# First token blocks' low parts moved to GpSimd and eight steps later, and three smaller moves around them

## The reference

```
# q, k, v: (4 batches, 8 heads, 576 rows, 64)
scores = q @ k.T / 8, masked where row//64 < column//64
x = softmax(scores) @ v                    # as 2304 tokens x 512
x = (sigmoid(x @ w_gate) * (x @ w_val)) @ w_out      # 512 -> 1536 -> 512
p = domain_probs / (domain_probs.sum(-1) + 1e-9)
out = sum over e of p[:, e] * (relu(x @ w1[e]) @ w2[e])   # 4 experts, 512 -> 1024 -> 512
```

## Time and profile before

| | |
|---|---|
| median of 3 runs | 1469.93 us (1467.77 to 1473.21) |
| the profiled execution | 1468.38 us |
| its span | 1466.6 us |
| busy: TensorE, VectorE, ScalarE, GpSimd | 1418.0, 905.8, 728.5, 424.0 us |
| scores of step 0 begin | 14.36 us |
| last steps' row maxima | up to 281 us |

### The profile page before, as it was taken

How to read it: one execution, slowest core, us unless ns; L and a number is a source line. 1 busy time by engine, 2 the same in 40 slices (tenths; PEclk the granted TensorE clock), 3 DMA queues, 4 the chain that set the end, 5 groups by cost and what they waited for, 6 DMA issues and landing times.

```text
span 1466.6 us, 22252 instructions
## 1 busy us (share of the span) xinstructions
PE 1418.0 (97%) x7816; PEld 1288.6 (88%) x7816; DVE 905.8 (62%) x1557; ACT 728.5 (50%) x1472; POOL 424.0 (29%) x665
## 2 busy tenths in 40 slices
PE   6999988899999999999999999999999999999999
PEld 4777776799998989898999989899899999899897
DVE  4888879777646446376774546364857746364453
ACT  4878777666434334254663534253546535253341
POOL 3656655544302122021441112021134312021200
PEclk9999999999999999999999999999999999999999
DMA  7787797223214121122223132131222322131302
GB/s 177 182 205 179 188 225 174 60 66 87 81 35 144 44 86 59 57 87 86 65 81 100 60 100 65 51 95 45 77 87 72 98 61 72 44 101 43 97 12 79
DMA packets 201150, 136.76 MB, mean 93 GB/s; under 512 B 66096, under 2 KB 170576, under 8 KB 201040
## 3 DMA queue, kind: packets, MB, share of 16 engines
q1 hardware_dynamic: 200976, 135.31, 33.2%
q0 software_dynamic: 64, 0.04, 0.1%
HBM read 97.55 MB, written 9.44 MB: 73 GB/s over the span
## 4 chain that ended last, share of the span: by engine, by line
PE 84%; DVE 8%; DMA 2%; issue 2%; ACT 1%; SPq 1%; POOL 1%; ACTq 0%; DVEq 0%; POOLq 0%
PE pb L903 26%; PE pb L905 25%; PE pb L904 25%; PE pt L395 3%; PE ov L420 2%; DVE ptl L330 2%; DVE nmax L308 1%; PE st L432 1%; PE st L383 1%; DMA craw<-in_moe_w_dram 1%; PE st L384 1%; DVE x1p L343 1%; DMA xb<-x1d 1%; DVE qtl L336 1%; DVE ktl L336 1%
## 5 line engine op out<-in xcount | busy, mean ns | idle before, releaser
L903 PE MATMUL pb<-xch,ul 128*128 128x384 f32 x1176 | 398.9, 339 | 5.7 <-DVE cb L837 4.2
L905 PE MATMUL pb<-xch,uh 128*128 128x384 f32 x1176 | 393.5, 335 | 0.0
L904 PE MATMUL pb<-xcl,uh 128*128 128x384 f32 x1176 | 393.3, 334 | 0.0
L697 POOL TENSOR_TENSOR us<-ura 128x256 f32<-128x256 f32 x84 | 62.3, 742 | 851.4 <-DVE ul L659 833.2
L903 PEld LDWEIGHTS pb<-xch,ul 128*128 128x128 f32 x1176 | 220.7, 188 | 23.8 <-issue 16.7
L905 PE MATMUL pb<-ch,rh 128*128 128x512 f32 x576 | 224.6, 390 | 0.0
L904 PE MATMUL pb<-cl,rh 128*128 128x512 f32 x576 | 224.5, 390 | 0.0
L903 PE MATMUL pb<-ch,rl 128*128 128x512 f32 x576 | 224.0, 389 | 0.0
L904 PEld LDWEIGHTS pb<-xcl,uh 128*128 128x128 f32 x1176 | 220.9, 188 | 0.4
L905 PEld LDWEIGHTS pb<-xch,uh 128*128 128x128 f32 x1176 | 220.7, 188 | 0.0
L806 DVE TENSOR_TENSOR cl<-craw,ch 128x512 fp32r<-128x512 f32 x132 | 92.0, 710 | 114.4 <-ACT ch L741 114.0
(11 more groups left out here) (99 smaller groups left out, 2558.2 us busy)
## 6 DMA issues: line engine op xcount, KB each, us to landing
ura<-in_moe_w_dram SPq DMA_DIRECT2D x96, 256.0 KB, 3.1
craw<-in_moe_w_dram SPq DMA_DIRECT2D x96, 256.0 KB, 2.8
ura<-in_moe_w_gate_dram SPq DMA_DIRECT2D x36, 256.0 KB, 3.2
ura<-in_moe_w_val_dram SPq DMA_DIRECT2D x36, 256.0 KB, 3.2
craw<-in_moe_w_out_dram SPq DMA_DIRECT2D x36, 256.0 KB, 3.1
qhl<-qth SPq DMA_DIRECT2D x32, 144.0 KB, 2.7
qhl<-qtl SPq DMA_DIRECT2D x32, 144.0 KB, 2.6
qlh<-qtl SPq DMA_DIRECT2D x32, 144.0 KB, 2.6
```

Of the source, the lines that this page charges most:

```text
L697: nc.gpsimd.tensor_tensor(us[:, 0, :], a21, a22, ALU.add).then_inc(us_ok, 1)
L903: nc.tensor.matmul(acc, lhs[1], rhs[0], start=start, stop=False, skip_group_check=True)
L904: nc.tensor.matmul(acc, lhs[0], rhs[1], start=False, stop=False, skip_group_check=True)
L905: return nc.tensor.matmul(acc, lhs[0], rhs[0], start=False, stop=stop, skip_group_check=True)
```

## The change

Four things change, all inside the attention's span.

1. At the start, ScalarE and no longer SyncE issues the loads of k's first pair and the four stacked copies of k for pair 0.
2. The four GpSimd sums of weight units 0 and 1 stand in four steps (58 to 61, 78 to 81) and no longer all in step 60 or 80; `lo_s` for these two units becomes two operations of 512 columns, in steps 69 and 70, 87 and 88.
3. The token blocks' sums and high parts of f = 0 begin eight steps later (wait for xb in step 122 and no longer 114).
4. The 14 low parts of f = 0 are made by GpSimd (steps 126 to 149) and no longer by VectorE. Two of VectorE's in-place sums in each column half now wait for x_lo, the count of low parts made, before they overwrite a block (`sum_t`, i = 0 and 2).

In the diff, functions that only get an `eng` argument are left out (`load`, `stack`, `stack_k`, `x_minus`, `lo_b11`, `lo_t1`, `lo_b22`, `lo_t`; `x_dve_b21` becomes `lo_b21`).

```diff
 @block.sync
-            load(0, q_v, qn, q_in)
-            load(0, k_v, kn, k_in)
-            load(0, v_v, vn, v_in)
+            load(sp, 0, q_v, qn, q_in)
+            load(sp, 0, v_v, vn, v_in)
             next_q(0)
+            sp.wait_ge(prep_lo, 1)
             for h in range(2):
-                sp.wait_ge(prep_lo, 1)
                 stack_q(0, h)
-                sp.wait_ge(prep_lo, 2)
-                stack_k(0, h)
             next_k(0)
 @block.scalar
+            load(act, 0, k_v, kn, k_in)
             for p in range(2):
                 prep(p)
+            act.wait_ge(prep_lo, 2)
+            for h in range(2):
+                stack_k(act, 0, h)
             for t in range(STEPS + TAIL):
...
         def sum_t(f, c, i):
             if i == 0:
+                if f == 0:
+                    dve.wait_ge(x_lo, 2 * c + 1)
                 nc.vector.tensor_tensor(block_of(c, 0, 0), block_of(c, 1, 1), xt[:, c, :], ALU.subtract)\
...
             if i == 2:
                 dve.wait_ge(x_sum, XSUMS * f + 2 + 3 * c + 1)
+                if f == 0:
+                    dve.wait_ge(x_lo, 4 + 5 * c + 1)
                 nc.vector.tensor_tensor(block_of(c, 1, 0), block_of(c, 1, 0), block_of(c, 0, 0), ALU.subtract)\
...
+        def lo_s_half(n, m):
+            r = n % 2
+            at = slice(3 + 2 * m, 5 + 2 * m)
+            dve.wait_ge(ws_hi, n + 1)
+            lo = nc.vector.tensor_tensor(ul[r][:, at, :, :]..., us[:, 2 * m:2 * m + 2, :]..., uh[r][:, at, :, :]..., ALU.subtract)
+            if m == 1:
+                lo.then_inc(ws_lo, 1)
...
         def with_pool(pool, t):
-            if t == 60:
-                sums_of_weights(pool, 0)
+            if t in (58, 59, 60, 61):
+                sum_of_weights(pool, 0, t - 58)
...
+            if t in (126, 130):
+                lo_b11(pool, 0, (t - 126) // 4)
+            if t in (128, 132):
+                lo_t1(pool, 0, (t - 128) // 4)
+            for c in range(2):
+                first = 133 + 9 * c
+                if t == first:
+                    lo_b21(pool, 0, c)
+                if t == first + 2:
+                    lo_t(pool, 0, c, 0)
+                if t == first + 3:
+                    lo_b22(pool, 0, c)
+                if t in (first + 5, first + 7):
+                    lo_t(pool, 0, c, (t - first - 3) // 2)
         def with_act(act, t, qk_ps):
-            if t in (116, 118):
-                hi_b11(0, (t - 116) // 2)
+            if t in (123, 125):
+                hi_b11(0, (t - 123) // 2)
...
         def with_dve(dve, t, qk_ps):
-            if t in (114, 115):
-                sum_t1(0, t - 114)
+            if t in (122, 123):
+                sum_t1(0, t - 122)
...
+                if t == 129 + 8 * c:
+                    sum_t(0, c, 0)
+                if t == 130 + 8 * c:
+                    sum_t(0, c, 1)
+                if t == 135 + 9 * c:
+                    sum_t(0, c, 2)
```

More of the change, by code:

```diff
@@ L134, in x1_head, with load, stack @@
             return x1p[64 * (g % 2):64 * (g % 2) + 64, g // 2 % X1_RING, :]
+        def load(eng, n, src, dst, got):
+            for h in range(2):
+                eng.dma_start(dst[:, 0:4, h, :], src[2 * n + h, 0:4 * P, :]
+                              .rearrange("(t p) d -> p t d", p=P)).then_inc(got, 16)
+            eng.dma_start(dst[0:S - 4 * P, 4, :, :],
+                          src[2 * n:2 * n + 2, 4 * P:S, :].rearrange("a p d -> p a d")).then_inc(got, 16)
+        def stack(eng, moves, h, got):
+            for dst, at, src in moves:
+                dst = dst[at:at + 64, h, FRAME - S:FRAME] if dst.shape[2] == FRAME else dst[at:at + 64, h, :]
+                eng.dma_start(dst.bitcast(F32), src[64 * h:64 * h + 64, :].bitcast(F32)).then_inc(got, 16)
@@ L136, in _, with stack_k @@
+        def stack_k(eng, u, h):
+            stack(eng, ((khl[u], 0, kth), (khl[u], 64, ktl)), h, k_stacked[u][h])
         @block.sync
         def _(sp):
[L138 to L148, removed]
             def stack_q(u, h):
-                stack(((qhl[u], 0, qth), (qhl[u], 64, qtl), (qlh[u], 0, qtl), (qlh[u], 64, qth)), h, q_stacked[u][h])
-            def stack_k(u, h):
-                stack(((khl[u], 0, kth), (khl[u], 64, ktl)), h, k_stacked[u][h])
+                stack(sp, ((qhl[u], 0, qth), (qhl[u], 64, qtl), (qlh[u], 0, qtl), (qlh[u], 64, qth)), h,
+                      q_stacked[u][h])
@@ L156, in next_q @@
             def next_q(n):
                 sp.wait_ge(prep_ps, 2 * n + 1)
-                load(n + 1, q_v, qn, q_in)
+                load(sp, n + 1, q_v, qn, q_in)
             def next_k(n):
                 sp.wait_ge(prep_ps, 2 * n + 2)
-                load(n + 1, k_v, kn, k_in)
+                load(sp, n + 1, k_v, kn, k_in)
             def pair_out(n):
@@ L179, in pair @@
                 for h in range(2):
-                    stack_k(n % 2, h)
+                    stack_k(sp, n % 2, h)
                 after(sp, v_lo, CHUNKS * n)
-                load(n, v_v, vn, v_in)
+                load(sp, n, v_v, vn, v_in)
                 if not last:
@@ L620, in x_dve_rest @@
                 sum_t(f, c, i)
[L621 to L624, removed]
+            lo_t(dve, f, c, 0)
+            lo_b22(dve, f, c)
+            lo_t(dve, f, c, 1)
+            lo_t(dve, f, c, 2)
         def hi_a(act, n):
@@ L688, in load_xb, with sum_of_weights @@
             sp.dma_start(xb[:, :, :], x1d[:, :, SUPER * s:SUPER * s + SUPER]).then_inc(xb_in, 16)
-        def sums_of_weights(pool, n):
+        def sum_of_weights(pool, n, i):
             r = n % 2
[L692 to L702, removed]
+            a11, a12, a21, a22 = (ura[r][:, m, :] for m in range(4))
+            if i == 0:
+                pool.wait_ge(u_in[r], 32 * (n // 2 + 1))
+                if n:
+                    pool.wait_ge(ws_lo, n)
+                pool.sem_inc(pool_on, 1)
+                nc.gpsimd.tensor_tensor(us[:, 0, :], a21, a22, ALU.add).then_inc(us_ok, 1)
+            if i == 1:
+                nc.gpsimd.tensor_tensor(us[:, 2, :], a11, a21, ALU.subtract).then_inc(us_ok, 1)
+            if i == 2:
+                pool.wait_ge(us_ok, 4 * n + 1)
+                nc.gpsimd.tensor_tensor(us[:, 1, :], us[:, 0, :], a11, ALU.subtract).then_inc(us_ok, 1)
+            if i == 3:
+                pool.wait_ge(us_ok, 4 * n + 3)
+                nc.gpsimd.tensor_tensor(us[:, 3, :], a12, us[:, 1, :], ALU.subtract).then_inc(us_ok, 1)
         later = ExitStack()
@@ L1058, in with_act @@
                     hi_b22(0, c)
-                if t in (first + 5, first + 6, first + 7):
-                    hi_t(0, c, t - first - 5)
+                if t == 131 + 10 * c:
+                    hi_t(0, c, 0)
+                if t == 132 + 10 * c:
+                    hi_t(0, c, 1)
+                if t == 138 + 8 * c:
+                    hi_t(0, c, 2)
             k = t - STEPS
@@ L1212, in _ @@
             for n in range(2, UNITS * SUPERS):
-                sums_of_weights(pool, n)
+                for i in range(4):
+                    sum_of_weights(pool, n, i)
         @block.scalar
```

83 lines of the change are left out of this document (36 added, 47 removed).

## The result

The changed kernel takes 1475.11 us in the median of 12 runs (1474.09 to 1479.3), the kernel before 1470.2 of 12. The ratio is 1.0036 (95% interval 1.0025 to 1.0047): 5.3 us slower, where 1465, with 1457 to 1471, had been forecast. The profiled execution took 1479.3 (span 1477.5), 4.2 above the median and the slowest of the twelve, so that its waits can be longer than those of a usual one. TensorE's first product of the next stage starts at 292.50 instead of 283.13; what comes after takes 1.5 us more, in code that is the same. That part takes 1181.6 to 1186.5 us in the profiles of all versions here, so 1.5 us of it say nothing.

What follows compares the result with a forecast made beforehand. TensorE and VectorE, handing each other work in a ring, were taken to bound the attention, TensorE alone what follows. Start 1.2, weight sums 1.5 and token blocks 1.1 took 3.8 us off 1468.4; forecast 1465, range 1457 to 1471.

Steps and rivals of the forecast that it cites:

- eight steps are 12.2 us, so this wait goes: Token blocks: starting eight steps later ends VectorE's 3.49 us wait for the xb load.
- terms 4 to 6: Token blocks: VectorE's remaining sums cost 1.3 and 0.9 us, ScalarE's roundings 0.6, GpSimd and VectorE holding each other up 0.8.
- The start: Before the first score: ScalarE issuing k's loads and copies wins 1.2 us, ends nothing and 2.1; SyncE's issues set the time.
- rival C: Start: k's loads delay q's first load and the DMA engines are the limit; 0 instead of 1.2, 1466 us; chance 0.12.
- The weight sums: Steps 65 to 94: spread sums and halved subtractions win 1.5 us (0.5 to 2.5); other three halves and splits put at 2.5.
- step 70's 0.65: Weight units: the half subtraction at step 70, at a group's start where VectorE has no gap, costs its 0.65 us.
- The two new waits: Token blocks, steps 135 and 144: VectorE waits 3.2 and 4.4 us for GpSimd's low parts, 0.94 already a gap; sum 6.7.
- GpSimd's price: Token blocks: one low part of 384 columns takes GpSimd about 0.95 us, ends 0.73 and 1.46.
- The clock: Token blocks: the granted clock falls after each of two new waits, 1.3 us each, 2.6 together.
- The signs: VectorE waiting some 3 us at steps 135 and 144, clock 0.5 after each, no xb wait, first score 13.2, low parts 0.95.
- Rival A: Token blocks: low parts at 0.73, two waits of 2.0 us, clock stays; 6.4 won there, 1459 us; chance 0.26.
- Rival B: Steps 130 to 149: GpSimd becomes the bound and normalisations come late; 10 us lost there, 1476 us; chance 0.08.

Runs made afterwards that it cites:

- a_late: Changed kernel with VectorE's third sums three steps later, other second-half sums and ScalarE's roundings shifted too, GpSimd's work unchanged: 1464.65 us, ratio 0.9967.
- a_lows_dve: Changed kernel with the 14 low parts moved back from GpSimd to VectorE at the same steps: 1470.63 us, ratio 1.0003.
- a_late_early: Changed kernel with VectorE's sums later and three quarters of the xb load issued in four earlier pieces: 1460.61 us, ratio 0.9941.
- b_start: Kernel before with the start alone changed, ScalarE issuing k's first loads and stacked copies: 1470.63 us, ratio 0.9997.
- b_copies: Kernel before with only k's four stacked copies issued by ScalarE, k's loads staying on SyncE: 1468.09 us, ratio 0.9993.
- a_split: Changed kernel with the xb load in two halves, both behind q's load of pair 13: 1474.02 us, ratio 1.0028.
- b_weights: Kernel before with the weight units alone changed, one GpSimd sum per step and the subtraction in halves: 1469.89 us, ratio 0.9992.
- lows_dve_split: Changed kernel with low parts on VectorE at the same steps and the xb load in two halves behind q's: 1463.92 us, ratio 0.9953.

## Why the prediction was wrong

- **The step that failed**: "eight steps are 12.2 us, so this wait goes." VectorE's wait did; the time did not. The same load had put the DMA engines behind, and what was late next was q of pair 13: group 115 took 14.73, 7.1 above 7.65, where the forecast had nothing. Rows that showed it were there: the DMA share of 1.02 in the earlier trace rows. The forecast said which wait ends and not what is late behind it on the same queue. Moving the consumer of a late load uncovered another that queues behind the load. In a_late and a_lows_dve, with the same code up to there, the group took 12.11 and 13.30, so the 7.1 is 4.5 to 7.1 by execution. The groups of steps 110 and 115 together took 20.30 us in the kernel before and 19.80 (a_late), 21.00 (a_lows_dve) and 22.42 (the changed kernel) with the later consumer: one wait was exchanged for the other. Of the 5.0 us that the forecast took off there (20.30 less two groups of 7.65), 0.5 came at best, and in the changed kernel's profile 2.1 were lost. a_late_early shows the cause: with the load spread out the group takes 7.61.
- **The rest of the blocks.** With 7.1 taken off, steps 110 to 149 are 76.2, against a forecast of 61.2 + 12.9 = 74.1. The six groups from step 120 on take 60.86, 15.0 over 45.9: the waits 7.24, the clock 2.8 and 4.9 left, where terms 4 to 6 (VectorE's sums, ScalarE's roundings, the two engines holding each other up) had 3.6. They were set too low together; which of them was isn't shown.
- **The start**, 1.2: gave nothing (b_start 0.9997). It was the term's own lower end and rival C; b_copies shows that its reason, that the time is spent in SyncE's issues, was false. What a start is worth at step 15 can't be read from one trace: with the changed start that step begins between 38.74 (a_late) and 41.30 us (a_split).
- **The weight sums**, 1.5: 0.3 in the stretch, within what the same code differs by. The mis-sized term is the 2.5 for the other three halves and splits; step 70's 0.65 was named (0.7 measured).
- **The two new waits**, 3.2 + 4.4 = 7.6, or 6.7 with the old gap taken off: 7.24 measured. **GpSimd's price**, 0.95: 1.004. **The clock**, 2.6: 2.8 by a_late. These steps were right, and their chain stands in the trace: rinv at 242.44, GpSimd's normalisation at 244.47 and low part at 245.07, VectorE's sum at 246.17. The low parts' move loses 4.9 by itself.
- **The signs** that had been named came true all but one (the waits at steps 135 and 144, a clock of 0.50 behind each, no wait for xb, low parts of 1.0 us; the first score came at 14.95 and not at 13.2), and the time was still outside. None of them looked at q.
- **Rival A** took it that gaps of about 1 us leave the clock whole. The kernel before has one of 0.94 us, at 31.5, with the clock at 0.50 behind it (last section).
- **Rival B** had the right side and the wrong cause: GpSimd was busy for 90% of steps 135 to 149 in a_late, and they took 25.29 us, less than the 27.54 to 28.01 with the low parts on VectorE. The rival of a late transfer was missing among those that end slower.
- 5.3 us slower is then: GpSimd's part 4.9 (shown by a_lows_dve), the start, the weights and the eight later steps together about 0.4, since the later steps only exchanged a wait of VectorE for one of TensorE.

## What to carry to other kernels

When work that waits for a large load is moved later, ask what else is queued behind that load, and whose need comes first now. Spread such a load over time as soon as its parts are ready; here its order in the queue only chose who waits. When work goes to a slower engine, the place of its consumer has to be counted from that engine's own releases: here sums two or three steps later made 10 us of difference, between a loss and a gain.

## What the runs showed of the hardware that was not expected

- The same wait of TensorE at step 41 (1.85 or 1.86 us, for VectorE's ptl) brought a fall of the granted clock in some executions and not in others: that group takes 10.87 or 10.88 in the kernel before and b_start, 9.60 in b_weights and 9.58 in the changed kernel, the code there being the same. 1.3 us hang on it.
- Issuing from two engines of the core did not add transfer: with k's copies issued by ScalarE (b_copies), a stacked copy of the first 14 us takes 3.5 to 4.6 us to land instead of 2.6 to 2.9, and the first score is not earlier.
- A wait of 1.86 us in lows_dve_split left the clock at 1.00; one of 2.58 in a_split let it fall to 0.50 for about 7 us.
- So the length of one wait does not tell whether the clock falls. TensorE at step 10 in the kernel before, and its stretch of 34 to 35 us:

```profile
31.51 0.30 PE L395 MATMUL pt<-ident,probs 128*128 128x128 f32 x1 [0.94 <-DVE ptl L330]
...
34.00:35.00 1.00, 1.00 (x5) 0.58 (x5) 0.32 (x1) 0.98 (x3) 0.92 (x3) 0.50 0.77 180
```

and in a_late, with the same wait and no fall:

```profile
32.26 0.30 PE L397 MATMUL pt<-ident,probs 128*128 128x128 f32 x1 [0.94 <-DVE ptl L332]
...
34.00:35.00 1.00, 1.00 (x8) 0.78 (x7) 0.92 (x3) 0.86 (x4) 0.21 (x1) 1.00 0.62 134
```
